# Memory-cell attention, gated FFN and routed experts in one kernel: W_in split by 128 columns, q and phi in one load, hand-over reordered, padding's x columns zeroed in the last tile

## What is computed

```python
a = softmax(phi, over the 576 positions)             # per batch, head, memory cell
k_m = a^T k;  v_m = a^T v                            # 32 cells of 64
attn = softmax(q k_m^T / 8) v_m                      # (8, 8, 576, 64)
x = attn laid out as (4608 tokens, 512)
h = x @ w_in;  x = (h * sigmoid(1.702 h)) @ w_out    # dense FFN
logits = x @ w_gate;  e = argmax(logits);  gate_w = softmax(logits)[e]
eom = sigmoid(x @ w_output_gate)
out[token] = gate_w * eom[e] * (relu(x @ w1[e]) @ w2[e])
```

## Time and profile before

| | us |
|---|---|
| median of 3 runs | 1329.37 |
| the profiled execution, its own time | 1328.66 |
| its span (first to last instruction) | 1327.0 |
| TensorE busy | 1306.9 (98%) |
| GpSimd, VectorE, ScalarE busy | 564.8, 624.0, 389.5 |
| DMA moved | 274.20 MB, 207 GB/s over the span |

### The profile page before, as it was taken

One profiled execution on the slowest core, in us unless ns is written; L12 is line 12 of the kernel. 1 busy time (PEld: TensorE's weight loads), 2 busy tenths in 40 slices (PEclk: granted clock), 3 DMA queues, 4 the chain that ended last, 5 costly groups with the idle time before them and its releaser, 6 DMA issues.

```text
span 1327.0 us, 23583 instructions
## 1 busy us (share of the span) xinstructions
PE 1306.9 (98%) x6876; PEld 1052.2 (79%) x6877; DVE 624.0 (47%) x1281; ACT 389.5 (29%) x722; POOL 564.8 (43%) x666
## 2 busy tenths in 40 slices
PE   7999999999999999999999999999999999999998
PEld 4557888888888888888888888887888888888886
DVE  4884333533433435334344343347655555555553
ACT  4773222222322222223222222233222222222221
POOL 2778944433433543344334343412343342433332
PEclk9999999999999999999999999999999999999999
DMA  9999466565465554654655546647873789548882
GB/s 383 406 391 323 150 203 192 187 180 186 165 194 182 189 176 159 179 192 155 193 182 171 177 175 176 196 162 234 245 227 100 217 247 251 164 134 261 240 246 76
DMA packets 154507, 274.20 MB, mean 207 GB/s; under 512 B 17427, under 2 KB 54676, under 8 KB 152148
## 3 DMA queue, kind: packets, MB, share of 16 engines
q1 hardware_dynamic: 97764, 203.21, 44.8%
q10 hardware_dynamic: 43728, 38.55, 11.9%
q0 software_dynamic: 12960, 31.72, 7.5%
HBM read 144.92 MB, written 100.45 MB: 185 GB/s over the span
## 4 chain that ended last, share of the span: by engine, by line
PE 93%; DMA 4%; DVE 1%; ACT 1%; issue 0%; POOL 0%; ACTq 0%; SPq 0%; POOLq 0%; DVEq 0%
PE ps L808 29%; PE ps L776 29%; PE ps L849 16%; PE ps L878 16%; DMA kvm<-in_kv 3%; PE ps L818 1%; PE ps L695 1%; DMA phT<-in_phi 0%; PE ps L676 0%; PE ps L744 0%; PE ps L668 0%; ACTq L1113 0%; POOL sc L1677 0%; ACT aT L958 0%; PE ps L709 0%
## 5 line engine op out<-in xcount | busy, mean ns | idle before, releaser
L776 PE MATMUL ps<-xs,W 128*128 (+1 forms) x1728 | 417.7, 390 | 0.9 <-DVE gate L1306 0.9
L808 PE MATMUL ps<-W,gs 128*128 128x512 f32 x1728 | 414.8, 389 | 0.1
L776 PEld LDWEIGHTS ps<-xs,W 128*128 128x128 f32 x1728 | 322.9, 188 | 70.6 <-issue 2.7
L808 PEld LDWEIGHTS ps<-W,gs 128*128 128x128 f32 x1728 | 324.3, 188 | 67.7 <-DVE gs L1311 0.5
L1306 DVE TENSOR_TENSOR gate<-ps,gate 128x512 f32<-128x512 f32 x144 | 99.6, 692 | 361.7 <-ACT gate L1048 361.4
L1048 ACT ACTIVATE gate<-ps 128x512 f32<-128x512 f32 x144 | 86.2, 598 | 462.3 <-PE ps L776 444.8
L1736 POOL CAST whi<-raw 128x512 fp32r<-128x512 f32 x128 | 84.5, 660 | 321.6 <-DMA raw<-in_moe_w 321.6
L878 PE MATMUL ps<-W,chT 128*128 (+1 forms) x936 | 218.1, 389 | 1.4 <-DVE chT L1473 1.4
L849 PE MATMUL ps<-W,cx 128*128 (+1 forms) x936 | 218.8, 390 | 0.3 <-issue 0.3
L878 PEld LDWEIGHTS ps<-W,chT 128*128 128x128 f32 x936 | 175.6, 188 | 38.3 <-issue 1.8
L849 PEld LDWEIGHTS ps<-W,cx 128*128 128x128 f32 x936 | 175.4, 188 | 37.2 <-issue 0.9
(11 more groups left out here) (163 smaller groups left out, 783.1 us busy)
## 6 DMA issues: line engine op xcount, KB each, us to landing
W<-expert_scratch SPq DMA_DIRECT2D x24, 2048.0 KB, 11.2
raw<-in_moe_w SPq DMA_DIRECT2D x128, 256.0 KB, 2.8
expert_scratch<-whi SPq DMA_DIRECT2D x128, 256.0 KB, 2.7
expert_scratch<-raw SPq DMA_DIRECT2D x128, 256.0 KB, 3.0
cq<-ch ACTq DMA_DIRECT2D x156, 128.0 KB
kvm<-in_kv SPq DMA_DIRECT2D x15, 1152.0 KB, 12.6
crec<-record_scratch POOLq DMA_DIRECT2D x160, 64.0 KB
qT<-in_q SPq DMA_DIRECT2D x16, 576.0 KB, 12.1
```

The costliest lines, as they stand in the source:

```text
L776: mm = pe.matmul(ps[:, f % 2, :], W[:, col:col + P], xs[:, bass.ds(x0 + (x_lo * K1 + c) * T, T)], start=(c == 0 and w_lo + x_lo == 0), sto ...
L808: mm = pe.matmul(ps[:, 2 + s, :], gs[:, f % 2, g_lo, s * P:(s + 1) * P], w_out_sb[:, f, w_lo, :], start=(f == 0 and g_lo + w_lo == 0), sto ...
```

## The change

- W_in is laid out so that one piece of 256 KB is one chunk f: all 512 rows by 128 columns. `w_order` gives the order of the 32 pieces: in 0 to 3, out 0 and 1, in 4, out 2 and 3, then in and out by turns. Two pieces (`AHEAD = (9, 10)`) are loaded and split within stage A instead of four; mm1(0, f) waits for its own piece.
- q and phi become one array: row g holds q(g) and phi(g+2). Groups 0 to 12 load both at once; phi(0), phi(1) and phi(15) come alone. The joint load waits for `s_sc` at g-2 and also for `s_aT` at g, which only phi's load did before.
- Hand-over: VectorE takes the last group's maximum at once (the low part of x's last row block goes to GpSimd), ScalarE runs the last exponential before the first sigmoid, so one table load is left of three. TensorE's mm1(0,0) takes that low part last.
- `pad` stores 12 columns of 524. The 512 x columns are zeroed ahead by `fill`: in the last tile, right after the first expert's number is read, SP stores 9 x 128 rows of zeros in each of the eight regions, from the place where tile 6 ended. GpSimd waits for all of them (`b_fill`) before it scatters tile 7's records.
- ScalarE makes the high part of h of block 1 before it moves h of block 2.

```diff
+            if width > QA * D:
+                wait(sp, s_aT, g)
+            sp.dma_start(qph[g % 3][:, 0:width], qphi[g * P:(g + 1) * P, 0:width]).then_inc(s_q[g % 3], 16)
@@
-        QUARTER = (5, 6, 9, 10)
+        AHEAD = (9, 10)
@@ def pad
-            eng.dma_start(rec_dram[bass.ds(end, P), :], padrec[:]).then_inc(b_pad, 16)
+            eng.dma_start(rec_dram[bass.ds(end, P), DM:REC], padrec[:, DM:REC]).then_inc(b_pad, 16)
+        OPEN = 2 * SUB + 1
+        def fill(eng, e):
+            end = eng.value_load(tbl[0:1, 7, NE + e:NE + e + 1], min_val=e * REGION, max_val=e * REGION + N - 2 * T)
+            eng.dma_start(rec_dram[bass.ds(end, OPEN * P), 0:DM].rearrange("(j p) d -> p j d", p=P),
+                          padrec[:, 0:DM].rearrange("p (o d) -> p o d", o=1).broadcast_to([P, OPEN, DM])).then_inc(b_fill, 16)
@@ SP, after the tiles
             sp.wait_ge(b_first, 1)
             first_e = sp.value_load(tbl[0:1, 6, 0:1], min_val=0, max_val=NE - 1)
+            for e in range(NE):
+                fill(sp, e)
             sp.wait_ge(b_h, (NT - 1) * C1 + C1 // 2)
             load_expert(first_e, 0, range(2))
@@ TensorE, mm1
-                if isinstance(t, int) and t == 0 and f % 4 == 0:
-                    pe.wait_ge(s_wlo, n_in(K1 - 1, f // 4) + 1)
+                if isinstance(t, int) and t == 0:
+                    pe.wait_ge(s_wlo, n_in(f) + 1)
@@ ScalarE, hand-over
+            exp_scores(NG - 1, 1)
             g_sigmoid(0, 0)
-            exp_scores(NG - 1, 1)
             x_out(NG - 3, 1)
@@ ScalarE, stage C
+            act_h_hi(1, 1)
             act_h_move(2, 0)
-            act_h_hi(1, 1)
             act_y(0, 0)
@@ VectorE, hand-over
             scores_in(NG - 1, 1)
-            dve.wait_ge(b_xhi, 2)
-            dve.tensor_tensor(xs[:, (2 * K1 - 1) * T:2 * K1 * T], kept(K1 - 1), xs[:, (K1 - 1) * T:K1 * T].bitcast(F32),
-                              ALU.subtract).then_inc(s_x3, 1)
-            inverses(NG - 2)
             scores_max(NG - 1, 1)
@@ GpSimd, block of the last tile
+                    if i == 4 and last:
+                        pool.wait_ge(b_fill, 16 * NE)
                     if i == 4 and not first:
                         scatter_records(t - 1)
```

More of the change, by code:

```diff
@@ L465, in load_x, with load_phi @@
                 sp.dma_start(xraw, xT_rows[:, :, bass.ds(t * T, T)]).then_inc(b_xraw, 16)
-            def load_phi(g):
-                wait(sp, s_aT, g - 2)
-                sp.dma_start(phT[g % 3][:], phi[g * P:(g + 1) * P, :]).then_inc(s_phi[g % 3], 16)
+            def load_phi(g, row):
+                wait(sp, s_aT, g - 1)
+                sp.dma_start(phT[phi_slot(g)], qphi[row * P:(row + 1) * P, QA * D:QA * D + S]).then_inc(s_phi[g], 16)
             def load_kv(g):
@@ L486, in store_kept, with load_w @@
                              keep_v[:, :, kept_at(b, u):kept_at(b + n, u)]).then_inc(stored, 16)
-            def load_w(n, src):
-                if n in (K1 + 2, K1 + 3):
+            def load_w(n):
+                if n in (2, 3):
                     sp.wait_ge(s_kv, NG - 1)
                 else:
[L493 to L500, removed]
+                    wait(sp, s_wlo, n - 3)
+                kind, f = w_order[n]
+                sp.dma_start(w_raw[n % 4], w_in_v[f] if kind == "in" else w_out_v[f]).then_inc(s_wraw[n % 4], 16)
+            load_phi(0, NG - 2)
             sp.dma_start(ident[:], cst["ident"]).then_inc(s_cst, 16)
-            load_phi(1)
+            load_phi(1, NG - 1)
             load_q(0)
-            load_phi(2)
             for g in range(1, NG):
                 load_kv(g)
[L508 to L527, removed]
+                load_q(g, QA * D + (S if g < NG - 3 else 0))
+                if g == NG - 3:
+                    load_phi(NG - 1, g)
+                if g in AHEAD:
+                    load_w(AHEAD.index(g))
+            for n in range(2, 6):
+                load_w(n)
             store_kept(0, FIRST, 0, s_xu0)
@@ L565, in sp_tile @@
                     load_x(t + 1)
-                    load_w_out(5)
+                    load_w(11)
                     store_kept(2, 1, 1, s_xu1)
[L568 to L572, removed]
+                    for b in range(3, KEPT):
+                        load_w(9 + b)
+                        store_kept(b, 1, 1, s_xu1)
+                    load_w(16)
+                    load_w(17)
                     for dst, src in ((region, "region"), (iota8, "iota8"), (token, "token")):
@@ L768, in mm1 @@
                 x0 = (t % 2) * (2 * K1 * T)
-                if isinstance(t, int) and t == 0 and f % 4 == 0:
-                    pe.wait_ge(s_wlo, n_in(K1 - 1, f // 4) + 1)
+                if isinstance(t, int) and t == 0:
+                    pe.wait_ge(s_wlo, n_in(f) + 1)
                 for c in range(K1):
-                    if first:
+                    lo_last = first and c == K1 - 1
+                    if lo_last:
+                        pe.wait_ge(b_xhi, 2)
+                    elif first:
                         pe.wait_ge(b_xlo, c + 1)
-                    for w_lo, x_lo in ((0, 0), (0, 1), (1, 0)):
+                    for w_lo, x_lo in ((0, 0), (1, 0), (0, 1)) if lo_last else ((0, 0), (0, 1), (1, 0)):
+                        if lo_last and x_lo:
+                            pe.wait_ge(b_xlo, K1)
                         col = f * FW + (w_lo * K1 + c) * P
@@ L777, in mm1 @@
                                        xs[:, bass.ds(x0 + (x_lo * K1 + c) * T, T)],
-                                       start=(c == 0 and w_lo + x_lo == 0), stop=(c == K1 - 1 and w_lo == 1))
+                                       start=(c == 0 and w_lo + x_lo == 0), stop=(c == K1 - 1 and (x_lo if lo_last else w_lo) == 1))
                 mm.then_inc(b_h, 1)
@@ L1823, in _ @@
             blocks(pool, pool_block, pool_drain)
-_INS = ["q", "kv", "phi", "moe_w_in", "moe_w_out", "gates", "moe2_w1", "moe2_w2"]
+_INS = ["qphi", "kv", "moe_w_in", "moe_w_out", "gates", "moe2_w1", "moe2_w2"]
 def lay_out(inputs):
@@ L1845, in lay_out @@
     gates = np.stack([by_row, by_block], 1).reshape(P, 4 * K1 * NE)
-    return {**inputs, "q": q, "kv": kv, "phi": phi, "gates": gates}
+    w_in = inputs["moe_w_in"].reshape(K1, P, C1, P).transpose(2, 1, 0, 3).reshape(C1 * P, K1 * P)
+    return {**inputs, "moe_w_in": w_in, "qphi": qphi, "kv": kv, "gates": gates}
 def kernel(**inputs):
```

142 lines of the change are left out of this document (69 added, 73 removed).

## The result

The changed kernel takes **1362.6 us** (median of 4 runs, 1358.66 to 1363.56) against 1329.02 for the kernel before (4 runs): ratio 1.0245, with the interval 1.0232 to 1.0258. (Ratios and intervals in this document are worked out from all runs of both kernels, so they can differ a little from the quotient of the medians.) It is slower, and by 4.0 us more than was forecast: 1358.6, from 1352 to 1371. The profiled execution took 1363.56 us; its span is 34.9 us longer than that of before (1327.0).

What follows compares the result with a forecast made beforehand. Bytes bound the kernel until the hand-over, matmuls afterwards. From 1328.66: stage A -1.1, hand-over -0.85, fills +30.5, clock +1.7, after the stall -0.3, giving 1358.6 us, range 1352 to 1371.

Steps and rivals of the forecast that it cites:

- The mechanism and its size: Last tile: fills ahead of W1 in SP's queue delay stage C's first product, +30.5 us (+28 to +37); chance 0.80.
- The page's rule: Fills: HBM limit of about 358 GB/s per core would make them 52.7 us, the sum 3.5 us higher; not used.
- Stage A: Start to hand-over: fewer W_in bytes -1.24, merged q and phi loads -1.1, DMA gap +1.2; in sum -1.1 us.
- the hole: Start of stage A: joint load waits for an exponential, DMA queue runs empty near 17 us, +1.2 us (+0.5 to +2.5).
- Hand-over: Between stage A and the first tile: TensorE's waits of 0.16 and 0.91 us go, net -0.85 us (-1.1 to 0).
- the rival of the starving tile: First tile: just-in-time W_in pieces come late, TensorE waits +8 us, 1366 us with the stall; chance 0.06.
- Clock: Stage C's start: TensorE restarts at the half clock after 30 us idle, +1.7 us (0 to 2).
- After the stall: Stage C: W2 has 3 us of cover, pad costs 0, ScalarE's reordering gives -0.3 us (-1.4 to +0.5).
- ScalarE's swap: Stage C, high part of block 1 before block 2's move: removes a 1.43 us wait, block 2's product waits instead, -0.3 us.
- The fills didn't hide: Rival, last tile: W1's loads don't stand behind the fills, so only the gains are left, 1325.3 us; chance 0.06.
- half rate: Rival, last tile: gapped 2048 B rows store at about 200 GB/s, fills take 94 us, 1403 us; chance 0.08.

Runs made afterwards that it cites:

- both repairs: Changed kernel without the fills, q(1) and q(2) loaded apart from phi, and h of block 2 moved before block 1's high part: 1326.36 us, ratio 0.9979.

## Why the prediction was right, point by point

**The mechanism and its size.** The place of the fills (where W1's first load was issued before), W1 standing behind them in the same queue, and the second W1 load issued only when the first had landed: these steps held. The prediction's positions are those of before's trace, and the changed kernel ends its last tile 1.30 us earlier (884.80 for 886.10), so they are to be read less 1.30. The fills, forecast from 853.7 to 904.7, were issued from 852.44 on and let the waiting scatter go at 907.02. W1 landed at 911.6 and 920.6 for 910.7 and 919.7, and the first product ran at 920.64 for 921.1, since the 1 to 2 us that the scatter was to add to W1 didn't come. The queue from 890 to 906 moved 2979 packets at a share of 1.058 of 16 engines:

```profile
q1 hardware_dynamic: 2979, 6.00, 105.8%
```

That is 16 x 16 x 1.058 / 2979 = 91 ns per packet of 2 KB against the 85.4 taken from the earlier trace rows. Here the forecast had luck. A share above 1 says that the times of packets overlap, so the price of the queue is better read as packets per microsecond: 193 in the earlier trace rows and 186 here. The prediction multiplied by the share of 1.031 and didn't divide by it again, which made its 49.2 us 3% too long, and the pace was 4% lower than in its row: 9216 packets at 186 per microsecond are 49.5 us. Part of the detail was wrong without harm: I had the W1 load issued at once behind the fills, but SP itself was held for 38 us. Had anything else stood on SP's program there, it would have been late as well.

**The page's rule.** In the windows of the fills the DMA engines moved 378 to 383 GB/s, all traffic together, and the slope of the run with five ninths is 399. The Trainium skill ("DMA: Bandwidth & Descriptors", Specifications) gives about 358 GB/s for a core; by that the sum would have been 3.5 us higher, and the measurement, 5% or more above that rate, decides against it. Its rule that descriptors are consumed in ring order ("Queues, rings and completion order") agrees with the 20.66 us of the first W1 load.

**Stage A: -0.62 for -1.1.** The term that was mis-sized is the hole. I priced it at 1.2 us with the queue empty at 17.1 and the next load issued at 17.03. In the changed kernel that load came later:

```profile
18.29 0.33 SPq L497 DMA_DIRECT2D qphT<-in_qphi  x1
```

The load waits for an exponential, and the exponential comes behind TensorE: in all twelve traces this load (in before, and where q is apart, that of phi alone) is issued 3.45 to 3.47 us after the end of six matmuls (L744 of before and after) that start at 8.4 to 9.7. How late they end differs between executions: they took 3.89 us in before, 5.20 in the changed kernel, 4.39 to 4.94 in the others. Why, I can't say; the clock granted over them doesn't order them (0.73 in before, 1.00 in the changed kernel). Eight traces have the joint load at the start, two have q apart; some of them:

| trace | load issued | DMA share 17 to 20 | last k/v product that waits |
|---|---|---|---|
| before | 17.03 | 1.05 | 81.99 |
| changed kernel | 18.29 | 0.24 | 81.37 |
| h of block 2 moved first | 17.89 | 0.35 | 80.98 |
| without the fills | 17.34 | 0.52 | 80.42 |
| W2 held back | 16.44 | 0.83 | 79.74 |
| q apart | 17.11 | 1.04 | 80.01 |
| both repairs | 16.82 | 1.04 | 79.59 |

With the joint load each microsecond that it is late costs 0.9 us at the end of stage A. The eight have a mean of 80.54 there, the two with q apart 79.80, before 81.99. So the savings in bytes and packets are there (2.2 us, where 2.34 were forecast for 13 joint loads and these two kernels have 11), the hole cost 1.6 us in the execution that was profiled for the changed kernel and 0.7 on the mean, and the -0.62 is the least that any of the eight gained. That one execution fell near the forecast says little. In before the same spread mattered little, since q(2) kept the queue full.

**Hand-over: -0.76 for -0.85.** In size as worked out. The next late one is GpSimd, as forecast, but earlier than forecast, at mm1(0,0)'s last matmul and with 0.21 us:

```profile
93.78 0.51 PE L781 MATMUL ps<-xs,W 128*128 128x512 f32 x1 [0.21 <-POOL xs L1701]
...
103.15 3.01 PE L781 MATMUL ps<-xs,W 128*128 128x512 f32 x12
```

The wait of 0.91 us before mm1(0,3) is gone, and no mm1 of the first tile waited for its piece of W_in: the rival of the starving tile didn't happen (+0.08 us from mm2(0,0) to the last tile).

**Clock: +2.5 for +1.7.** I took the 3 us of idle time at the start for the pattern and bounded the loss at 2. After 30 us idle the first product took 5.38 us where 2.88 is normal: it ran at half clock nearly throughout. What came behind it was at full clock again (the 16 transposes take 1.91 us in both kernels, the clock from 926 on is 1.00). The charge came from a window of 3.4 us at 0.55 with only 3.17 us of busy TensorE in it; no row of before shows a whole product at the half clock.

**After the stall: +3.95 for -0.3.** This is the step that failed; its upper bound was +2. I argued that W2 had 3 us of cover and that nothing else would be late. W2 was in time, if barely: its second load, issued at 930.10, took 12.0 us, for a use at 942.9. But h of the first block goes through DMAs to another layout, and the stall had pushed these onto that load. VectorE's first transpose of h, ended by that move:

```profile
942.54 1.30 DVE L1469 STREAM_TRANSPOSE cqT<-cq 128x512 f32<-128x512 f32 x2 [5.13 <-DMA cq<-ch]
```

Before, the same transpose waited 0.3 us at most. TensorE lost 2.97 us by it, then 0.92, and after this short idle time the clock fell again: 0.66 granted from 945 to 950. Of the 3.95 us, 2.2 are waits (2.97 + 0.92 against 1.43 + 0.27) and 1.8 are slower matmuls (the 72 of the first three products with W2 take 18.52 us against 16.75).

```profile
945.00:950.00 5.00, 4.17 (x11) 3.35 (x12) 4.66 (x19) 0.00 (x0) 0.00 (x0) 0.66 0.23 51
```

What makes the moves late is read from a comparison of traces and not shown by an experiment. The moves come soon after W2's second load, and the sooner, the longer TensorE waits before block 0's product with W2:

| trace | moves issued after W2's second load, us | TensorE's wait, us |
|---|---|---|
| TensorE kept busy | 0.2 | 3.69 |
| fills alone | 1.1 | 3.37 |
| changed kernel | 1.5 | 2.97 |
| five ninths of the fills | 2.0 | 2.02 |
| before; without the fills | 5.5; 5.6 | 0; 0 |
| W1 ahead of the fills | 15.6 | 0 |

The last tile's scatter can't be what differs: it starts 5.8 us after the moves in every one of them. What fits is W2's second load, in whose way the moves come. The run that held W2 back doesn't contradict this: there the moves came 5.4 us after W2's first load, with 0.37 us of wait on VectorE. ScalarE's swap, the only thing that I had put into this term, had the wrong sign as well: -0.3 was forecast, from a wait of 1.43 us traded for a shorter one, but the run that undoes the swap is faster, by 1.2 us at this place in its trace. (With both repairs together only 0.3 of that are left.)

**The rivals.** The fills didn't hide, they didn't run at half rate (186 packets per microsecond against 193, so the gap of 48 B between rows cost 4% at the most), and the first tile didn't starve. Narrow padding rows without any fill were not tried, because the x columns would then be unset.

In sum the forecast of 1358.6 was 5.0 us below the profiled execution (4.0 below the median). Of these 5.0, the time behind the stall gives 4.25, the clock 0.8 and stage A 0.5; the stall itself was 0.5 shorter than forecast.

## What to carry to other kernels

A DMA that is "early" in the text is as early as its engine gets there: look up when the queue's engine ends what stands before it, and then what stands behind the new bytes. Here 18.9 MB were put ahead of loads that TensorE needed 39 us later (853 to 892 in before), to shorten a store of 2.1 MB that was not due for 54 us (906.99). A large store often has two gates, its place in the queue and the wait for its end; moving it past one shows the other, so price both. And a load that is joined to another inherits the later of both waits: where the queue is the bound, a hole at the start (0.7 us on the mean) costs more than the packets that the first two joint loads save (0.2 us by the prediction's 11 ns). A single profiled execution can stand at the edge of what a stage does from one execution to the next, so a term of a few tenths of a microsecond needs several traces.

## What the runs showed of the hardware

- SP was held while it issued to a full queue: eight stores of 2.4 MB took 38.34 us to issue, where eight of 262 KB took 11.30.
- With stores of 2048 B rows with gaps of 48 B the DMA engines moved 378 to 383 GB/s, 186 packets per microsecond, against 193 in the earlier trace rows.
- After 30 us idle TensorE's clock was at 0.50 and cost 2.5 us on the first 12 matmuls. After the short wait of 2.97 us it was 0.66 from 945 to 950.
- Moves of h that were issued 0.2 to 2.0 us after a load of 2 MB came so late that TensorE waited 3.69 to 2.02 us; issued 5.5 us or more after it, TensorE did not wait for them.
- The same six matmuls at the start (L744) took 3.89 to 5.20 us in twelve traces, and the load that waits behind them came at 16.44 to 18.29 us. A change that makes the DMA queue depend on the start is exposed to that.
